# A 64-point transform with its phase factors moved into the matrices around it, and the loads around it moved forward

## The reference

```python
batch, seq, d_model = (4, 5696, 128)      # x: (4, 5696, 128), h: (5696, 128)

def _attn_ref(x, h) -> np.ndarray:
    B, S, D = x.shape
    L = 2 * S
    Xf = np.fft.rfft(x, n=L, axis=1)
    Hf = np.fft.rfft(h, n=L, axis=0)
    Yf = Xf * Hf[None, :, :]
    y = np.fft.irfft(Yf, n=L, axis=1)[:, :S, :]
    return y.astype(np.float32)

def reference(...):
    x = attn_out.reshape(B * S, D)        # 22784 tokens of 128
    x = _moe_ref(x=x, **moe_kwargs)       # 8 experts of fixed capacity, greedy assignment
    return _moe2_ref(x=x, **moe2_kwargs)  # 8 experts, top 1, gated
```

## Time and profile before

| what | value |
|---|---|
| median of 3 runs | 2297.41 us (2294.53 to 2301.22) |
| the profiled execution's own time | 2292.75 us |
| its span | 2290.9 us |
| mean granted TensorE clock | 0.926 of full speed |
| busy share of the span | PE 85%, DVE 55%, ACT 41%, POOL 31% |
| stage 1, first to last matmul | 10.9 to about 192 us |
| stage 2, first to last matmul | 206.9 to 438.4 us |
| stage 3, first matmul to last group | 451.9 to 622.4 us |
| the two mixtures of experts | the rest, to 2290.9 us |

### The profile page before, as it was taken

One profiled execution on the slowest core, in us unless ns is written; L12 is line 12 of the kernel. 1 busy time (PEld: TensorE's weight loads), 2 busy tenths in 40 slices (PEclk: granted clock), 3 DMA queues, 4 the chain that ended last, 5 costly groups with the idle time before them and its releaser, 6 DMA issues.

```text
span 2290.9 us, 34896 instructions
## 1 busy us (share of the span) xinstructions
PE 1936.3 (85%) x10057; PEld 1490.5 (65%) x10057; DVE 1268.5 (55%) x4025; ACT 949.8 (41%) x2046; POOL 716.5 (31%) x618
## 2 busy tenths in 40 slices
PE   7786898699913889787879797978779999999998
PEld 3343444355511667666666666766579999999998
DVE  2223777522376676666666666411346666666665
ACT  2333787522121333333333333433335555555554
POOL 0001000000043435353535454545414344444434
PEclk9998999899955899998999999988989999999999
DMA  6876999777685011111110101101178888888885
GB/s 185 256 239 219 306 309 312 243 193 203 182 312 187 23 36 30 40 30 41 29 43 27 45 27 45 47 29 35 40 264 280 282 278 283 280 281 283 278 283 171
DMA packets 161012, 382.26 MB, mean 167 GB/s; under 512 B 29813, under 2 KB 88876, under 8 KB 135581
## 3 DMA queue, kind: packets, MB, share of 16 engines
q1 hardware_dynamic: 120749, 287.59, 39.5%
q10 hardware_dynamic: 11696, 57.94, 7.3%
q0 software_dynamic: 28480, 35.66, 5.4%
HBM read 273.07 MB, written 109.13 MB: 167 GB/s over the span
## 4 chain that ended last, share of the span: by engine, by line
PE 56%; issue 15%; POOL 9%; DMA 9%; DVE 7%; SPq 2%; ACT 1%; another core or an unknown queue 1%; ACTq 0%; POOLq 0%; DVEq 0%
PE bank L951 8%; PE bank L952 8%; PE bank L953 8%; POOL sorted L1659 5%; PE bank L864 5%; DMA arena<-in_dft_mid_dram 4%; POOL xr L1650 4%; PE bank L767 3%; PE bank L768 2%; DMA arena<-in_h_dram 2%; PE bank L688 2%; PE bank L689 2%; PE bank L788 2%; DVE ge L1395 2%; PE bank L887 2%
## 5 line engine op out<-in xcount | busy, mean ns | idle before, releaser
L1154 ACT ACTIVATE arena<-bank 128x356 f32<-128x356 f32 x512 | 238.9, 469 | 525.1 <-PE bank L887 413.4
L1553 DVE SCALAR_TENSOR_TENSOR hlo<-bank,hhi 128x374 fp32r<-128x374 f32 x544 | 297.8, 548 | 191.3 <-ACT hhi L1187 137.1
L864 PE MATMUL bank<-arena 128*128 128x356 f32 x1024 | 402.5, 476 | 0.0
L1187 ACT ACTIVATE hhi<-bank 128x374 fp32r<-128x374 f32 x544 | 262.9, 483 | 251.4 <-PE bank L953 209.5
L1687 POOL DMA_INDIRECT out_dram<-orow,slot x204 | 247.0, 1211 | 381.4 <-DVE slot L1592 323.7
L1650 POOL DMA_INDIRECT xr<-conv_y,idx x192 | 211.3, 1101 | 202.1 <-PE bank L828 133.8
L885 PE MATMUL bank<-xhi,wsp 128*128 128x356 f32 x512 | 258.1, 504 | 12.4 <-issue 5.2
L1659 POOL DMA_INDIRECT sorted<-arena,slot x192 | 194.2, 1011 | 143.9 <-DVE slot L1332 82.4
L951 PE MATMUL bank<-xhi,wsp 128*128 128x374 f32 x544 | 193.2, 355 | 3.0 <-DMA wsp<-w_split 3.0
L864 PEld LDWEIGHTS bank<-arena 128*128 128x128 f32 x1024 | 186.3, 195 | 0.7
L1631 POOL TENSOR_TENSOR wsp<-arena,wsp 128x1024 fp32r<-128x1024 f32 x16 | 40.8, 2551 | 464.2 <-ACT wsp L1104 464.2
(11 more groups left out here) (216 smaller groups left out, 3693.8 us busy)
## 6 DMA issues: line engine op xcount, KB each, us to landing
wsp<-w_split SPq DMA_DIRECT2D x136, 1024.0 KB, 5.4
arena<-spec_a SPq DMA_DIRECT2D x90, 320.0 KB, 3.4
spec_a<-arena ACTq DMA_DIRECT2D x16, 1600.0 KB
spec_b<-arena SPq DMA_DIRECT2D x90, 256.0 KB, 3.5
arena<-spec_b SPq DMA_DIRECT2D x16, 1280.0 KB
arena<-in_dft_mid_dram SPq DMA_DIRECT2D x90, 192.0 KB, 4.3
arena<-in_moe_w_dram SPq DMA_DIRECT2D x32, 512.0 KB, 6.3
w_split<-wsp ACTq DMA_DIRECT2D x16, 1024.0 KB, 5.7
```

The source lines that it names most:

```text
L864: r = mm(bank[Z1[t % 2]][:, 0:T1], w2raw[u][:, f * D:(f + 1) * D], h32[:, f, :], start=(f == 0), stop=(f == FC - 1))
L1154: nc.scalar.activation(h32[:, f, :], bank[H1[q % len(H1)]][:, 0:T1], ACT.Relu).then_inc(m_hh[0], 1)
L1187: nc.scalar.activation(hh[:, f, 0:T], bank[f % 4][:, 0:T], ACT.Relu).then_inc(m_hh[m_], 1)
L1553: v.scalar_tensor_tensor(hl[:, f, 0:T], bank[f % 4][:, 0:T], 0.0, hh.bitcast(F32)[:, f, 0:T], ALU.max, ALU.subtract).then_inc(m_hl[m_], 1)
```

## The change

The phase factors that stand between the transform of length 178 and the one of length 64 are no longer in the matrix of stage 2. They stand in the matrices of stage 1 and stage 3, which thereby become different for each of the 64 units; the matrix of stage 2 becomes the same for all 90 frequencies.

- `dft_fwd1` is now 96 x 64 x 2 x 90; each group loads its part (96 x 720 values) with its x, as a fifth DMA. `dft_inv1` is 96 x 64 x 2 x 89; each group of stage 3 loads 96 x 712 values. `dft_mid` is one matrix of 128 x 384, loaded once.
- Stage 1 has four buffers of x and `fwd1` (XB = 4) and three of `aout` (AB = 3). The buffers of stages 1 and 2 no longer lie over each other.
- The first six frequencies of stage 2 are loaded in two parts: the rows of groups 0 to 13 once these are stored, the rows of groups 14 and 15 at the end. Later ones are loaded once the forward matmul of unit k - 6 is done.
- Before the end of stage 2, ACT issues the load of partitions 0 to 79 of the first group of stage 3 (after unit 86's copies), and after its last copy that of the second group (`early_z`).
- Stages 1 and 2 are written out on all engines, without hardware loops.

```diff
+XB, AB = 4, 3
+NEAR = 14
+KEARLY = 80
...
-    ph = 2 * np.pi * ((n2 * kk + R1 * n2 * k2) % L) / L
+    a = 2 * np.pi * ((n1 * R2 + m2) * k1 % L) / L
...
+    ph = 2 * np.pi * (n2 * k2 % R2) / R2
...
+            xin = [cv(f"xin{i}", B + 1, G * D) for i in range(XB)]
+            fwd1 = [cv(f"fwd1{i}", G, 2, K1) for i in range(XB)]
+            aout = [cv(f"aout{i}", 2, G, SEQH) for i in range(AB)]
+            mid = cv("mid", MID)
...
+            def load_x(g):
+                u = g % XB
+                if g >= XB:
+                    sp.wait_ge(s1_h, G * (g - XB + 1))
                 for a, b in split(N1):
...
+                sp.dma_start(fwd1[u][0:KP, :, :, :], fwd1_d[:, G * g:G * (g + 1), :, :]).then_inc(x_ld[u], 16)
...
+            for g0, g1 in ((0, NEAR), (NEAR, NG)):
+                stored(g1)
+                for k in range(NB2):
+                    for r in range(2):
+                        sp.dma_start(a_in[k][R2 * r + G * g0:R2 * r + G * g1, :], a_d[k, r, G * g0:G * g1, :]).then_inc(a_ld[k], 16)
...
-                    if not isinstance(i, int):
-                        sp.wait_ge(s2_z, k - NB2 + 1)
-                    sp.dma_start(a_in[u][:, :], avk[bass.ds(k, 1)].rearrange("k p s -> (k p) s")).then_inc(a_ld[u], 16)
-                    sp.dma_start(m_in[u][:, :], mid_d[bass.ds(k, 1)].rearrange("k p s -> (k p) s")).then_inc(a_ld[u], 16)
-                    if u == NB2 - 1 or not isinstance(i, int):
-                        store_z(k - (NB2 - 1), u + 1)
...
+            for k in range(K1):
+                if k + NB2 < K1:
+                    sp.wait_ge(s2_x, k + 1)
+                    sp.dma_start(a_in[k % NB2][:, :], avk[k + NB2:k + NB2 + 1].rearrange("k p s -> (k p) s")).then_inc(a_ld[k % NB2], 16)
+                if k >= 3:
+                    store_z(k - 3)
...
-                for a, b in split(K1):
+                for a, b in ((KEARLY, K1),) if isinstance(i, int) else ((0, KEARLY), (KEARLY, K1)):
                     sp.dma_start(zin[u].rearrange("p r n s -> p r (n s)")[a:b],
                                  bv[a:b, :, bass.ds(g * (G * SEQ), G * SEQ)]).then_inc(z_ld[u], 16)
+                if not isinstance(i, int):
+                    sp.dma_start(inv1[u][0:KP, :, :, :], inv1_d[:, bass.ds(g * G, G), :, :]).then_inc(z_ld[u], 16)
...
+            def early_z(g):
+                bv = b_d.rearrange("k r n s -> k r (n s)")
+                act.wait_ge(s_zpad, 2)
+                act.dma_start(inv1[g][0:KP, :, :, :], inv1_d[:, G * g:G * (g + 1), :, :]).then_inc(z_ld[g], 16)
+                act.dma_start(zin[g].rearrange("p r n s -> p r (n s)")[0:KEARLY],
+                              bv[0:KEARLY, :, G * SEQ * g:G * SEQ * (g + 1)]).then_inc(z_ld[g], 16)
...
+                if k - 3 == KEARLY + 3:
+                    early_z(0)
             for k in range(K1 - 3, K1):
-                z_copy(k, k, k // 2)
+                z_copy(k)
+            early_z(1)
```

More of the change, by code:

```diff
@@ L255, in carve @@
                                **{k: d for k, d in zip(names, dims)})
[L257 to L271, removed]
+        inv1 = [carve(G, 2, N1) for _ in range(2)]
         zin = [carve(2, G, SEQ) for _ in range(2)]
-        assert at[0] <= stage1_end
         yout = [carve(B, G * D) for _ in range(2)]
@@ L727, in _, with stage2 @@
[L727 to L731 removed]
+                q = k % 2
+                mm(bank[6 + q][:, :], mid[:, 4 * R2:6 * R2], prod[q][:, 0, :], start=True, stop=True).then_inc(s2_z, 1)
+            def stage2(k):
+                u, q = k % NB2, k % 2
+                pe.wait_ge(a_ld[u], 64 + 16 * (k // NB2))
+                if k >= 2:
+                    pe.wait_ge(s2_hc, k - 1)
+                    pe.wait_ge(s2_mul, 2 * (k - 1))
+                hs = a_in[u][:, SEQ:SEQH]
+                for r in range(2):
+                    both = mid[:, 2 * r * R2:(2 * r + 2) * R2]
+                    last = mm(bank[2 + q][:, r * D:(r + 1) * D], both, hs, start=True, stop=True)
+                last.then_inc(s2_h, 1)
+                mm(bank[q][:, :], mid[:, R2:R2 + P], a_in[u][:, 0:SEQ], start=True, stop=True).then_inc(s2_x, 1)
+                if k >= 2:
+                    inverse2(k - 2)
@@ L734, in rows_T @@
+            pe.wait_ge(s_mid, 16)
+            pe.wait_ge(s1_act, R2)
+            pe.wait_ge(s1_dve, R2)
+            for k in range(K1):
+                stage2(k)
+            inverse2(K1 - 2)
+            inverse2(K1 - 1)
             def rows_T(t, u, m):
@@ L1076, in _ @@
-            stage2(0)
-            with act.Fori(1, K1 // NB2) as i:
-                stage2(i)
+            for t in range(R2):
+                g, m, q = t // G, t % G, t % 2
+                if m == 0 and g >= AB:
+                    act.wait_ge(a_st[g % AB], 32 * (g // AB))
+                act.wait_ge(s1_re, t + 1)
+                copy(aout[g % AB][0:K1, 0, m, 0:SEQ], bank[q][0:K1, :])
+                act.wait_ge(s1_h, t + 1)
+                copy(aout[g % AB][0:K1, :, m, SEQ:SEQH],
+                     bank[4 + q][0:K1, 0:2 * D].rearrange("p (r d) -> p r d", r=2)).then_inc(s1_act, 1)
+                if m == G - 1:
+                    store_a(g)
@@ new lines, in _ @@
+            for k in range(K1):
+                q = k % 2
+                act.wait_ge(s2_h, k + 1)
+                if k >= 2:
+                    act.wait_ge(s2_mul, 2 * (k - 1))
+                copy(hsp[q].rearrange("p r d -> p (r d)"), bank[2 + q][:, 0:2 * D]).then_inc(s2_hc, 1)
+                if k >= 3:
+                    z_copy(k - 3)
+                act.wait_ge(s2_x, k + 1)
+                copy(xri[q][0:R2, :], bank[q][R2:P, :])
+                copy(xri[q][R2:P, :], bank[q][0:R2, :]).then_inc(s2_xc, 1)
+                if k - 3 == KEARLY + 3:
+                    early_z(0)
```

281 lines of the change are left out of this document (106 added, 175 removed).

## The result

The changed kernel takes 2270.16 us (median of 4 runs, 2263.88 to 2279.9), the one before 2298.94 us beside it (4 runs): ratio 0.9881, 95% interval 0.9841 to 0.992. It is faster, but by half of what was forecast: 2240 us was predicted, and 2270 lies outside 2220 to 2262. Executions at a lower granted clock (5 of the 42 of kernels in which TensorE waits for `inv1` in stage 3, none of the other 70) are left out of the ratios, and of the two profiles among them (`store_first`, `s1_two_buffers`) the times are read up to where the clock falls.

A forecast was written before the change was run, and what follows sets the result against it. Late loads held stage 1, nearly full DMA stage 2, TensorE stage 3. Stage 1 -25.4, stage 2 -28.2, between stages 2 and 3 -4.5, stage 3 +1 summed to -57.1 us: 2240 us, range 2220 to 2262.

The forecast's parts named there:

- That round has 4.33 us ... it fits, at the slow end barely.: Stage 2: copy to `zout`, load issue and store landing were to fit into 4.33 us, so not hold the pace.
- waits of ACT's copy to `zout` for stores: Stage 2: listed sign that the forecast is wrong, ACT's copy waiting for stores of `spec_b`.
- The bound of the pace, 2.30: Stage 2: slow bound of the time per frequency, 2.30 us, if the `zout` round is late now and then.
- the pace of 2.165: Stage 2: additions every 2.165 us, set by the three compute engines; stage 200.2 instead of 231.5 us, -31.3 us.
- That the bytes set the old pace: Stage 2: removing 192 KB of 768 KB a frequency from a queue 91.8% busy leaves the pace to the compute engines.
- The term: Stage 1: limited by transfers at 0.97 occupancy with deeper buffers; stage 2 starts at 181.5 instead of 206.9, -25.4 us.
- The rival by which TensorE sets the pace: Stage 1: TensorE, not transfers, is the limit; stage 2 starts at 166, kernel 2225 us; chance 18%.
- The early loads: End of stage 2: `early_z(0)` costs +1.6 and +1.5 us; the way to stage 3 gets 4.5 us shorter.
- About 1 us in hand: Stage 3: each group's load with `inv1` fits with about 1 us to spare; +1 us for the first groups.
- the +14 that stood as the bound: Stage 3: upper bound of the cost, +14 us, if 14 groups are 1 us late.
- The rival of crowded transfers: Stages 1 and 3: competing loads and stores come late, +9.5 and +10 us; 2259 us; chance 24%.
- The code: Written-out stages 1 and 2: about 16 more instruction packets, given no cost in time.

The follow-up runs named there:

- store_first: Changed kernel with SP issuing each stage 2 store ahead of the load, two `zout` buffers kept: 2195.01 us beside 2201.46 for the kernel before.
- s1_two_buffers: Changed kernel with two buffers of x, `fwd1` and `aout` in stage 1, instead of four and three: ratio 1.0023 to the kernel before.
- z4: Changed kernel with four buffers of `zout` instead of two: 2142.31 us, ratio 0.9737 to the kernel before.
- z4_extra_loads: z4 with 192 KB more loaded for each frequency from the seventh on, for which TensorE waits: ratio 0.9744 to the kernel before.
- no_fwd_loads: Changed kernel loading `fwd1` for the first four groups only, later groups reusing those matrices: ratio 0.9834 to the kernel before.
- after_again: The changed kernel's same code, run and profiled again in another series: ratio 0.9901 to the kernel before.
- no_early: Changed kernel without early partial loads; SP loads stage 3's groups 0 and 1 whole behind the last stores: 2168.84 us beside 2201.46 before.
- z4_e1late: z4 with stage 3's group 1 loaded by SP behind group 0's last rows: ratio 0.9734 to the kernel before.
- inv_ring: Changed kernel with four buffers of `inv1`, each loaded a group ahead, behind that group's z: ratio 0.992 to the kernel before.
- combo: Changed kernel with the edits of z4, store_first, inv_ring and z4_e1late together: 2135.16 us, ratio 0.9694 to the kernel before.

## Why the prediction was wrong

**The step that failed: "That round has 4.33 us ... it fits, at the slow end barely."** The condition was seen and its price mis-sized, and waits of ACT's copy to `zout` for stores stood among the signs of being wrong. The sum was off as written: 0.59, 0.4 and 3.5 us are 4.49, which does not fit into 4.33. I took 2.0 to 3.5 us for the store to land, from the kernel before, and up to 0.4 us for the issue of the load. The round took 4.74 us, since the store lands after 4.1 us; store_first shows that the load directly ahead of it is 1.6 us of these. The bound of the pace, 2.30, came from "late now and then", where the whole stage turned on it: once the round is longer than two paces, every frequency pays. With z4 there are 194.0 us between the first and the last addition, 30.0 less than the 223.98 of the kernel before, against the 31.3 that I had worked out for the pace of 2.165; it keeps 2.180. So the compute pace was right; in the changed kernel the round (some 27 us) and the store delayed by the early load (some 5) took all of it.

**That the bytes set the old pace.** I read 91.8% in the earlier trace rows as the bound and the removed quarter as the cause of a gain. z4_extra_loads shows that this quarter can be loaded at no cost at 1.01 and 357 GB/s. In the old stage TensorE waited 19.1 us for loads that came late, but the queue was not at its ceiling: a busy share of 0.92 was none. That they came late because they were released late is argued, not shown.

**Stage 1: right in size, the reason open in part.** The term came out (-25.1 for -25.4; share 0.96 for the 0.97 taken, waits nearly gone), but a hit to 0.3 us is luck where the start moves from 173.3 to 181.8 us between profiles: -25 to -34. s1_two_buffers shows that the deeper buffers do it. That the transfers alone then bound the stage isn't shown: no_fwd_loads has 3.3 MB less to load and starts stage 2 no earlier than profiles with all loads. The rival by which TensorE sets the pace would have started it at 166; TensorE is near, at 98% busy in no_fwd_loads and after_again. The partial loads that I counted inside this term have no gain of their own that the runs show.

**The early loads: wrong in sign.** I gave `early_z(0)` 1.6 us for issues and 1.5 for its bytes. It made one store land 8.8 us after issue, on which ACT waited 5.08 us, and without the early loads (no_early) the stage is 6.1 us shorter. `early_z(1)` was weighed ("4.8 us of work") and then not charged: it takes 5.6 us of the boundary (z4 against z4_e1late). A rule of the Trainium skill bears on this ("DMA: Bandwidth & Descriptors", section "Issuing engines are not separate DMA queues"): DMAs of different issuing engines run on the same 16 DMA engines and interleave. The traces agree: a load issued by ACT, in a queue of its own, stood beside a store of SP that took 8.8 us to land, where the median is 4.1.

**Stage 3: the bound and not the value.** "About 1 us in hand" was not there; the matrix, issued last, lands 10.1 us after its issue, and pairs of groups take 22.15 us instead of 21.3. Of the +14 that stood as the bound, 7 came. The rival of crowded transfers was right here (+10) and wrong in stage 1.

**The code: right.** The packets of the two queues went from 43 and 44 to 52 and 51, 16 more as worked out, and the compute pace of 2.18 us in z4, written out in the same way with TensorE busy for 180.00 of 180.00 us, leaves no room for a stall.

**The rest,** +3.8 us of 1666, was put at nothing. It isn't the routing, which took 133.7 us before and 132.4 after; the first expert pass, which the change leaves alone, took 891.1 and 896.5 us. It moves by itself (below).

## What to carry to other kernels

Before giving a stage the pace of its engines, work out every buffer's round at that pace, with the landing time of its DMA behind what will stand ahead of it in the queue, and count it in full when it is longer. A store on which a buffer waits goes ahead of loads that have time; an early load of a megabyte in the other queue is paid by the stores that someone waits for. And a queue that is busy for 92% is not proved to be the bound: put the bytes back and see whether the pace moves.

## What the runs showed of the hardware

- **Share is not bytes.** z4 moves 269 GB/s at a share of 0.90, the kernel before 301 GB/s at 0.90, z4_extra_loads 357 at 1.01, all with the same queue. So a share near 1 does not tell how many bytes would still fit; why it doesn't, no run shows.
- **Order in a queue.** A 256 KB store lands 2.5 us after issue, and 4.1 us when a 320 KB load is issued 0.4 us ahead of it in the same queue.
- **VectorE and GpSimd in the routing.** One group of 15 comparisons takes 1.85 us in after_again and 3.99 us in inv_ring; beside it GpSimd's operation at that moment (timelines, after_again and then inv_ring):

```profile
637.85 1.85 DVE L1378 TENSOR_SCALAR ge<-qlow 128x178 bf16<-128x178 bf16 x15
```

```profile
639.11 2.78 POOL L1617 TENSOR_TENSOR wsp<-arena,wsp 128x1024 fp32r<-128x1024 f32 x1 [3.10 <-ACT wsp L1098]
```

```profile
638.07 3.99 DVE L1380 TENSOR_SCALAR ge<-qlow 128x178 bf16<-128x178 bf16 x15
```

```profile
638.12 2.35 POOL L1619 TENSOR_TENSOR wsp<-arena,wsp 128x1024 fp32r<-128x1024 f32 x1 [1.88 <-ACT wsp L1100]
```

  In inv_ring GpSimd starts inside the group, and the group is 2.14 us longer, about GpSimd's 2.35; in after_again GpSimd starts near the group's end and takes 0.43 us longer itself. Of the four groups between 625 and 664 us, three take 3.9 to 4.0 us in inv_ring, and one in after_again. The Trainium skill has a rule for it ("SBUF — State Buffer", section "SBUF: two separate sides"): an operation of GpSimd and one of VectorE that runs in a two-port mode, or has two inputs in SBUF, lock the pair of ports that they share for a whole instruction, and the other waits. These rows agree with it, but no row shows in which mode the comparisons run; no run here took GpSimd's work away, so that this moves the routing by 9 us is argued, not shown.
- **TensorE's clock.** In store_first, two windows of stage 3, columns as in the earlier trace rows:

```profile
520.00:530.00 10.00, 10.00 (x64) 5.94 (x63) 2.86 (x8) 2.32 (x4) 0.00 (x0) 1.00 0.84 199
540.00:550.00 10.00, 10.00 (x31) 5.25 (x31) 1.40 (x4) 1.16 (x2) 0.00 (x0) 0.50 0.52 130
```

  Between them TensorE was idle for 1.0 us, and then it stayed at half clock, 1.2 GHz, to the end of the stage, some 85 us, though busy throughout; that costs 40 us. s1_two_buffers has the same for 168 us. In both profiles the clock falls right behind the longest wait for `inv1` (timelines, store_first and then s1_two_buffers); behind their shorter waits for it the clock stays at 1.00:

```profile
535.63 1.12 PE L759 MATMUL bank<-arena 96*89 96x512 f32 x2 [0.99 <-DMA arena<-in_dft_inv_dram]
```

```profile
554.92 1.60 PE L759 MATMUL bank<-arena 96*89 96x512 f32 x2 [1.04 <-DMA arena<-in_dft_inv_dram]
```

  The kernel before has no such waits, and inv_ring and combo have none for `inv1`. That the loads added to stage 3 bring the half clock with them is argued from this, not shown; what holds it there is open.
- **The same kernel, 98 us apart.** The kernel before took 2197 to 2201 us in three series of runs and 2299 in two. The transform is alike in the profiles of both kinds of series; the difference lies in the first expert pass, which no kernel here changes: from its first to its last matmul of L856 (L864 before) 793 to 799 us in the one kind and 890 to 904 in the other, at a granted clock of 0.98 in after_again and 0.94 in the changed kernel's first profile. What differs isn't known.
